# Moving five score groups by a slot, giving GpSimd's low parts a count of their own, and sharing a block copy

## The reference

```python
def _attn_ref(q, k, v, alpha):
    for t in range(S):
        state = alpha[:, :, t, :, None] * state + np.einsum('bhd,bhe->bhde', k[:, :, t], v[:, :, t])
        y[:, :, t] = np.einsum('bhd,bhde->bhe', q[:, :, t], state)

def _moe_ref(x, w_in, w_out):          # 384 -> 2048 -> 384
    h = x @ w_in
    return (h - np.tanh(h)) @ w_out

def _moe2_ref(x, w_in, w_out, alpha):
    h = x @ w_in
    return (np.maximum(h, 0.0) + alpha * np.minimum(h, 0.0)) @ w_out
```

## Time and profile before

| what | value |
| --- | --- |
| median of three runs | 948.44 us (946.61 to 950.17) |
| the profiled execution | 944.54 us |
| its span, first to last instruction | 942.6 us |
| TensorE busy | 905.3 us, 96% |
| VectorE busy | 564.2 us, 60% |
| ScalarE busy | 327.2 us, 35% |
| GpSimd busy | 214.6 us, 23% |
| mean granted TensorE clock | 0.989 |

### The profile page before, as it was taken

How to read it: one execution, slowest core, us unless ns; L and a number is a source line. 1 busy time by engine, 2 the same in 40 slices (tenths; PEclk the granted TensorE clock), 3 DMA queues, 4 the chain that set the end, 5 groups by cost and what they waited for, 6 DMA issues and landing times.

```text
span 942.6 us, 22776 instructions
## 1 busy us (share of the span) xinstructions
PE 905.3 (96%) x9920; PEld 746.5 (79%) x9920; DVE 564.2 (60%) x710; ACT 327.2 (35%) x534; POOL 214.6 (23%) x196
## 2 busy tenths in 40 slices
PE   3788999999999999999999999999999999999998
PEld 3677788788788878877888888888888888888887
DVE  7778657764875686477534455555555555655553
ACT  6752633254335425332544441121211211212212
POOL 7654404331532244043304430000000000000000
PEclk8699999999999999999999999999999999999999
DMA  8550063026004500620045010010100100100000
GB/s 294 157 203 2 2 162 132 2 62 211 23 2 94 200 2 6 191 99 3 2 146 191 0 68 1 1 67 0 35 32 0 67 0 0 67 0 0 34 1 33
DMA packets 24965, 61.05 MB, mean 65 GB/s; under 512 B 3216, under 2 KB 11408, under 8 KB 22352
## 3 DMA queue, kind: packets, MB, share of 16 engines
q1 hardware_dynamic: 24880, 59.79, 20.4%
HBM read 46.15 MB, written 9.44 MB: 59 GB/s over the span
## 4 chain that ended last, share of the span: by engine, by line
PE 89%; DVE 4%; POOL 3%; issue 3%; ACT 0%; POOLq 0%; DVEq 0%
PE ph L716 40%; PE acc L725 14%; PE acc L726 13%; PE acc L727 13%; PE ps L536 4%; DVE q_w L977 2%; POOL k_t L1240 1%; PE ps L609 1%; PE py L609 1%; PE py L605 1%; POOL w_lo L1332 1%; PE ps L605 1%; DVE q_w L988 1%; DVE near L1010 1%; PE ps L530 1%
## 5 line engine op out<-in xcount | busy, mean ns | idle before, releaser
L925 ACT ACTIVATE g_hi<-g 128x512 fp32r<-128x512 f32 x192 | 121.2, 632 | 431.9 <-PE acc L727 335.7
L1161 DVE TENSOR_TENSOR g_lo<-g,g_hi 128x512 fp32r<-128x512 f32 x192 | 146.2, 762 | 187.5 <-ACT g_hi L925 186.4
L725 PE MATMUL acc<-g_lo,w_hi 128*128 128x512 f32 x576 | 226.4, 393 | 2.8 <-DVE g_lo L1161 2.8
L726 PE MATMUL acc<-g_hi,w_lo 128*128 128x512 f32 x576 | 224.3, 389 | 0.7 <-issue 0.7
L727 PE MATMUL acc<-g_hi,w_hi 128*128 128x512 f32 x576 | 224.2, 389 | 0.0
L716 PE MATMUL ph<-x_hi,w_lo 128*128 128x512 f32 x576 | 166.0, 396 | 0.9 <-DVE w_lo L1136 0.9
L716 PE MATMUL ph<-x_hi,w_hi 128*128 128x512 f32 x576 | 162.1, 390 | 0.0
L716 PE MATMUL ph<-x_lo,w_hi 128*128 128x512 f32 x576 | 162.0, 389 | 0.0
L725 PEld LDWEIGHTS acc<-g_lo,w_hi 128*128 128x128 f32 x576 | 108.1, 188 | 27.5 <-DVE g_lo L1161 4.8
L727 PEld LDWEIGHTS acc<-g_hi,w_hi 128*128 128x128 f32 x576 | 108.1, 188 | 23.7 <-issue 0.9
L716 PEld LDWEIGHTS ph<-x_hi,w_hi 128*128 128x128 f32 x576 | 108.1, 188 | 23.1
(11 more groups left out here) (139 smaller groups left out, 615.5 us busy)
## 6 DMA issues: line engine op xcount, KB each, us to landing
v_t<-v SPq DMA_DIRECT2D x6, 1024.0 KB, 6.3
a_t<-alpha SPq DMA_DIRECT2D x5, 1024.0 KB, 5.1
k_t<-k SPq DMA_DIRECT2D x5, 1024.0 KB, 6.9
x<-x_out SPq DMA_DIRECT2D x6, 768.0 KB, 8.0
x_in<-x SPq DMA_DIRECT2D x6, 768.0 KB, 4.9
kT<-trees SPq DMA_DIRECT2D x64, 64.0 KB, 2.0
q_w<-q SPq DMA_DIRECT2D x10, 384.0 KB, 5.6
out<-prob SPq DMA_DIRECT2D x5, 768.0 KB, 3.8
```

What stands on the lines that cost most here:

```text
L725: pe.matmul(acc[:, m, :], w_hi[:, f, part], g_lo[:, f % 2, :], start=(f == 0), stop=False)
L726: pe.matmul(acc[:, m, :], w_lo[:, f, part], g_hi[:, f % 2, :], start=False, stop=False)
L925: act.activation(g_hi[:, f % 2, :], g[:, f % 2, :], ACT.Copy).then_inc(g_hi_made, 1)
L1161: dve.tensor_tensor(g_lo[:, f % 2, :], g[:, f % 2, :], g_hi[:, f % 2, :].bitcast(F32), ALU.subtract).then_inc(g_lo_made, 1)
```

## The change

- `E_SLOTS`: in passes two to four groups 4, 5 and 6 move from slots 11, 14, 17 to 12, 15, 18, group 7 stays at 20, and group 8 moves from 23 to 22. In the first pass groups 4 to 8 move from 12, 14, 17, 20, 23 to 13, 16, 19, 21, 24; in pass five groups 4 to 7 move from 11, 14, 16, 19 to 12, 15, 17, 20 and group 8 stays at 22.
- Low parts: GpSimd makes slices 4, 5 and 6, with the count `w_lo_pool` of its own. VectorE makes all others, slice 3 too, now with 7 and 8 at slot 0 of the first pass. Slice 0 moves behind the far copies of lane 1, slice 1 behind the last `x_low`.
- Near blocks of lane 1: GpSimd copies the first two. VectorE copies the third ahead of its level-6 growth and the fourth ahead of the far copies, with the count `placed_vector`.
- `FILLING` is 4 instead of 5.

```diff
-E_SLOTS = {1: (3, 7, 12, 14, 17, 20, 23), 2: (3, 7, 11, 14, 17, 20, 23), 3: (3, 7, 11, 14, 17, 20, 23),
-           4: (3, 7, 11, 14, 17, 20, 23), 5: (3, 7, 11, 14, 16, 19, 22)}
+E_SLOTS = {1: (3, 7, 13, 16, 19, 21, 24), 2: (3, 7, 12, 15, 18, 20, 22), 3: (3, 7, 12, 15, 18, 20, 22),
+           4: (3, 7, 12, 15, 18, 20, 22), 5: (3, 7, 12, 15, 17, 20, 22)}
...
-FILLING = 5
+FILLING = 4
...
-W_LO_GPSIMD = 7
-W_LO_BESIDE = {0: [7], 1: [8], 2: [9, 10], 8: [11], 11: [12], 18: [13], 23: [14], 24: [15]}
+W_LO_GPSIMD = (4, 5, 6)
+W_LO_BESIDE = {0: [3, 7, 8], 1: [9], 2: [10], 9: [11], 11: [12], 18: [13], 23: [14], 24: [15]}
+W_LO_VECTOR = [f for f in range(NF) if f not in W_LO_GPSIMD]
...
# TensorE, first_y
-                pe.wait_ge(placed[lane], PLACED)
+                pe.wait_ge(placed[lane], PLACED if lane == 0 else PLACED // 2)
+                if lane == 1:
+                    pe.wait_ge(placed_vector, PLACED // 2)
# TensorE, layer, an "in" slot
-                    pe.wait_ge(w_lo_made, which * NF + f + 1)
+                    if which == 1:
+                        pe.wait_ge(w_lo_made, len(W_LO_VECTOR) + f + 1)
+                    elif f in W_LO_GPSIMD:
+                        pe.wait_ge(w_lo_pool, W_LO_GPSIMD.index(f) + 1)
+                    else:
+                        pe.wait_ge(w_lo_made, W_LO_VECTOR.index(f) + 1)
# VectorE
+            def place_near_first(lane, i):
+                dve.wait_ge(masked[lane], MASKED)
+                t = slice(NEAR * i, NEAR * i + NEAR)
+                heads = slice(DUO * H * lane, DUO * H * (lane + 1))
+                dve.tensor_copy(prob[t, heads, t], near[t, heads, :]).then_inc(placed_vector, 1)
...
                     if what == "level" and l == LEVELS and lane == 1:
-                        weights([0])
+                        place_near_first(lane, 3)
                         dve.wait_ge(scored[lane], l + 1)
...
                     if what == "Y" and (lane, l) == (0, 1):
+                        weights([0])
                         x_low(0)
                         x_low(1)
-                        weights([1])
...
                         if l == 1:
-                            weights(range(2, W_LO_FIRST))
+                            weights(range(1, W_LO_FIRST))
...
+                    if l == LEVELS - 1 and lane == 1:
+                        place_near_first(lane, 2)
...
-                    past(dve, w_lo_made, f)
+                    past(dve, w_lo_made, W_LO_VECTOR.index(f))
# GpSimd
-                for i in range(NB):
+                for i in range(NB // 2):
...
-            w_low(0, range(W_LO_FIRST, W_LO_GPSIMD))
+            for f in W_LO_GPSIMD:
+                w_low(0, f)
```

More of the change, by code:

```diff
@@ L289, in attention_mlp @@
         ld_w = [[sem(f"ld_w{which}_{f}") for f in range(NF)] for which in range(2)]
-        w_hi_made, w_lo_made = sem("w_hi_made"), sem("w_lo_made")
+        w_hi_made, w_lo_pool, w_lo_made = sem("w_hi_made"), sem("w_lo_pool"), sem("w_lo_made")
         scored, masked, copied = lanes_and_rest("scored"), lanes_and_rest("masked"), lanes_and_rest("copied")
-        placed = lanes_and_rest("placed")
+        placed, placed_vector = lanes_and_rest("placed"), sem("placed_vector")
         q_grown, k_grown, tree_made = lanes_and_rest("q_grown"), lanes_and_rest("k_grown"), lanes_and_rest("tree_made")
@@ L1092, in attention @@
                             if is_tile(a, 1):
-                                for lane in range(LANES):
-                                    dve.wait_ge(placed[lane], PLACED)
+                                dve.wait_ge(placed[0], PLACED)
+                                dve.wait_ge(placed[1], PLACED // 2)
+                                dve.wait_ge(placed_vector, PLACED // 2)
                         past(dve, masked[LANES], MASKED * n + i - 1)
@@ L1275, in first_tile @@
                         place_near_first(lane)
-                        pool.wait_ge(placed[lane], PLACED)
+                        pool.wait_ge(placed[lane], PLACED // 2)
                     if l < LEVELS:
@@ L1325, in attention, with w_low @@
                         pool.sem_inc(all_placed, 1)
[L1327 to L1333, removed]
+            def w_low(which, f):
+                pool.wait_ge(w_hi_made, which * NF + f + 1)
+                if which == 0:
+                    past(pool, w_lo_pool, W_LO_GPSIMD.index(f))
+                else:
+                    pool.wait_ge(w_lo_made, len(W_LO_VECTOR) + f)
+                pool.tensor_tensor(w_lo[:, f, :], raw(which, f), w_hi[:, f, :].bitcast(F32),
+                                   ALU.subtract).then_inc(w_lo_made if which else w_lo_pool, 1)
             pool.memset(ident[:, :], 0.0)
@@ L1360, in _ @@
             for h in range(HALF_SLOTS):
-                w_low(1, W_LAST.get(h, []))
+                for f in W_LAST.get(h, []):
+                    w_low(1, f)
 def kernel(q, k, v, alpha, moe_w_in, moe_w_out, moe2_w_in, moe2_w_out, moe2_alpha, moe_x=None, moe2_x=None):
```

## The result

The changed kernel takes 934.0 us in the median of six runs (933.17 to 936.59), the kernel before 947.53 us in six runs beside it (945.82 to 950.17). The ratio is 0.9861 (0.9841 to 0.9881), so 13.2 us are gained, with an interval from 11.3 to 15.1. The forecast was 8.7 us and a median of 939.7; the measured one lies 1.5 us under the low end of the range. The profiled execution took 936.59 us, 7.95 less than that of before.

The account below looks back on a forecast made before the run. TensorE's own work plus its stops was taken as the bound (busy 905.3 of 942.6 us). Gains of 3.9 + 0.9 + 2.7 + 1.2 = 8.7 us from the median 948.44 gave 939.7, range 935.5 to 945.

Parts of the forecast that it names:

- Group 4, passes two to five: Group 4 one slot later in passes two to five: TensorE's four waits for `near` go, 3.9 us gained.
- the thin place in front of group 8: Passes two to five: only two slots between groups 7 and 8, half a microsecond of cover for VectorE's growth, cost nothing.
- Rivals 3 and 4: 3: VectorE's late growth stops TensorE at group 8, about 943, chance 0.12; 4: near-wait moves to group 5, 943.6, 0.05.
- First pass: First pass, later slots: wait for slice 14 goes (0.9 us), and two code-fetch stops inside groups 4 and 5 (2.7).
- Rival 2: The stops in the first pass's groups stay in other places: 6.0 us gained, 942.4; chance 0.12.
- The near copies: Start: GpSimd copies two blocks instead of four; lane 1's first batch 0.7 us earlier, lost again by the third layer slot.
- The two counts: Start: VectorE's slice 7 no longer waits for GpSimd's four slices; TensorE's 2.84 us stop before the first "out" slot becomes 1.5.
- Gain taken: 1.2: Whole start: first "out" slot at 55.55 instead of 56.74, 1.2 us gained; bounds 3.8 gained and 0.7 lost.
- the worked chain: Start: GpSimd and VectorE steps blocking each other; slices 7 and 8 done at 54.9, first `g_lo` at 55.5.
- Rival 5: Start: thinner TensorE work brings the clock back only at 58.6 us, so slower, 954.8; chance 0.05.
- Rival 1: Start: no blocking between GpSimd and VectorE, all 3.8 us come, 937.1; chance 0.10.

Follow-up runs that it names:

- fill_36: The changed kernel with 32 more filling matmuls (FILLING 36 instead of 4): 946.37 us, ratio 1.0002 to the kernel before.
- fill_20: The changed kernel with 16 more filling matmuls (FILLING 20 instead of 4): 949.72 us, ratio 1.0026 to the kernel before.
- fill_68: The changed kernel with 64 more filling matmuls (FILLING 68 instead of 4): 939.21 us, ratio 0.991 to the kernel before.
- the two product runs: The changed kernel with GpSimd's first product of tile 1 waiting for the first `g_lo`, run twice: 932.27 and 932.28 us, ratios 0.9841 and 0.9848.
- the two timed runs: The kernel before with two counts, shared near blocks and FILLING 4: 942.91 us; with the two counts and their new order alone, FILLING 5: 943.13 us.
- the slots-only run: The kernel before with only the new slots of groups 4 to 8, in all passes: 938.55 us, ratio 0.9906.

## Why the prediction was too small

The traces give the terms apart. Each number is the distance between the starts of two layer slots in the timelines: from the first slot of pass one to its fourth "in" slot, from there to pass two, and over passes two to five. The runs with fill_36 and fill_20 are left out of every column but "to the fourth 'in' slot".

| kernels | start of the first slot | to the fourth "in" slot | rest of pass one | passes two to five |
| --- | --- | --- | --- | --- |
| old form, six traces, mean | 44.55 | 17.13 | 77.78 | 344.2 |
| new form, eight or nine traces, mean | 43.95 | 14.35 | 73.76 | 340.0 |
| difference | 0.6 | 2.8 | 4.0 | 4.2 |
| forecast | 0.7 | 0.5 | 3.6 | 3.9 |

(New form is: near blocks shared, without fill_68; two counts, without the two product runs; new slots in the last two. Old form is its opposite in each column.) The sum is 11.6 us, within 11.3 to 15.1, where 8.7 was forecast: 2.3 of the missing 2.9 are in the second column.

**Group 4, passes two to five: right.** All four near-waits go, none comes for groups 5 to 8, the second and third pass are 1.0 us shorter each, and the thin place in front of group 8 held. Rivals 3 and 4 did not happen. The timed gain of 5.3 is over the 4.2 of the traces, within its interval (4.0 to 6.6). Some of what is over 3.9 are stops at crossings, as one in `y_product` of pass four (0.67, 0.53 and 0.26 us in three of the old traces, in none with the new slots at this alignment); they vary too much from one execution to the next to be summed.

**First pass: right.** The two stops and the wait for slice 14 are gone, 3.6 us timed, 4.0 in the traces. Rival 2 did not happen. The rule of the Trainium skill ("Runtime: NRT & Kernel Launch", Instruction fetch mechanics) holds in its block of 256 instructions (126.5 matmul records, each with its weight load, are 253, and the waits come to it), and "mostly hidden" fails at some crossings, in dense groups of small matmuls above all: stops of up to 4.0 us. One sentence of the prediction was wrong: one filling matmul is two records with their weight loads, so four instructions and not two, and the added waits did not make up for it. The crossings stand two matmuls later in the program all the way (in pass four 119 of group 3's matmuls ahead of the cut instead of 117); it cost nothing that the runs could show.

**The near copies: right.** 0.6 at the first layer slot, nothing in the end. The copy took 0.42 us, as the 0.4 that was estimated from the Trainium skill's figures ("VectorE: DVE Perf Modes", The perf-mode tier table). GpSimd's product that began 0.04 us behind it took 1.29 us instead of 1.06. That it is held up agrees with the Trainium skill ("SBUF — State Buffer", Who interferes with whom); the 0.23 us more are less than the whole copy.

**The two counts: the term that was mis-sized.** The failed step is "Gain taken: 1.2", within it "VectorE then does slice 3 (51.1), waits for GpSimd's `a_t` product (1.9, to 53.0), does 7 and 8". It was taken as 1.2 us and measured 3.4 in the traces (0.6 and 2.8), 3.6 and 4.4 in the two timed runs. Of the 2.8, 1.9 are an earlier first out slot (12.65 us behind the first layer slot with one count, 10.80 with two, in the mean) and 0.9 the clock behind it. Two things took the place of the worked chain.

First, the `a_t` transfer landed at 52.6, 8.9 us after its issue, and not at 50.7, since it was issued at 43.68 and not 0.7 earlier and took a microsecond more (the 7.9 us of the earlier trace rows is the shortest of the six traces with one count, which go up to 9.1). So VectorE made its three slices unblocked by 52.85, 2.0 earlier than in the worked chain, and a different pair met: the product and the first `g_lo`. In seven of nine traces with two counts the product came first and TensorE stopped 0.8 to 1.3 us. In five of them it was the `g_lo` that took 2.38 us; in fill_36 and fill_20 the product met a slice ahead of it, which took 2.6, as in the prediction's chain. In two traces the product came second and nothing stopped. Both runs with the added wait, in which the `g_lo` took 0.69 and nothing stopped, show that this meeting is the cause.

Second, the old stop cost more than its 2.84 us. In four of the six traces with one count TensorE fell to 0.50, its 1.2 GHz level, for 3.4 us around the end of the stop; in the two traces of the kernel before it did not, and no trace with two counts shows it there. Three windows of the slots-only run, whose out slot began at 56.80 after 2.80 us idle, with the fields of the earlier trace rows:

```profile
50.00:56.60 6.60, 4.00 (x75) 3.21 (x73) 3.02 (x2) 1.85 (x3) 5.18 (x3) 1.00 0.79 300
56.70:60.00 3.30, 3.20 (x8) 2.52 (x9) 3.30 (x6) 1.23 (x2) 0.00 (x0) 0.50 0.98 357
60.10:66.00 5.90, 5.90 (x150) 4.79 (x149) 5.64 (x9) 3.52 (x4) 3.96 (x3) 1.00 0.29 106
```

From there TensorE reached its fourth "in" slot 17.5 to 18.0 us after the first, against 16.1 where the clock stayed up: 1.5 us more. The timed runs point the same way, weakly, since some of their means lack the first 40 us: the mean granted clock is 1.000 in 2 of the 67 runs of the kernel before beside the experiments, and in 5 of the changed kernel's 14. The prediction had summed against a single execution that was spared this. It had also come out near the fast end (944.54, where 30 runs beside one group of experiments lie between 944.04 and 951.25), and the profiled one of the changed kernel at the slow end, with a stop of 1.95 us and the half clock behind it in pass five; so the spans differ by 7.7 and the medians by 13.5. How much of the timed 13.2 over the traces' 11.6 is chance stays open. Rival 5, the clock at the start, did not happen: it was back at 41.4 us instead of 38.1, and the layers ran at full clock. Rival 1 was nearer than the forecast in size, but blocking was there: that its 3.8 us nearly came is luck, not its mechanism. The range's low end was also worked out wrong by 0.2 us (937.1 less 1.8 is 935.3, not 935.5); the measured 934.0 lies below either.

## What to carry to other kernels

When two engines fill one sequence under one count, look at how long each waits for the other's part. Here two counts, with one slice given to the other engine, brought about 4 us, and sharing a block copy nothing that could be timed. Price a stop of TensorE like this one (2.8 us) with the half clock that can come with it (1.5 us more here), and take the sum against several executions, since one profile can lack it. In an unrolled kernel with groups of a hundred or so small matmuls, the place of the code blocks is a quantity to be tried like any other, and an edit that shifts the instructions early in the stream has to be judged at several shifts.

## What was not expected of the hardware

- Sixteen or 32 filling matmuls at the start of TensorE's stream made the kernel 16 and 13 us slower, for the most part through crossings of code blocks (every 126.5 matmul records): single stops of 0.4 to 4.0 us, the long ones in or beside groups and batches of small matmuls. A whole block of filling cost only its own 5.7 us.
- Around the end of stops of 1.90 to 3.43 us TensorE was granted 0.50 for 3.4 us, and for 6.8 us with those of 2.72, 3.94 and 4.01 in the runs with more filling. It was not so at each: stops of 2.24 and twice 2.84 us left it at 1.00.
- VectorE's `g_lo` and GpSimd's `a_t` product do not run side by side: the `g_lo`, 0.68 us alone, took 2.38 where it began 0.13 us behind the product, and 0.68 where it began 0.15 us ahead of it.
